# A row of 8224 bytes instead of 8192 for the weights of each step, in a gated-product kernel in float32r

## What is computed

```python
kv = np.einsum('bhsd,bhse->bhde', k, v)             # batch 4, heads 8, seq 576, head 64
out = np.einsum('bhsd,bhde->bhse', q, kv)
x = out / sqrt(mean(out * out, -1) + 1e-6) * g_norm # then as 2304 tokens x 512
h = x @ w_in;  x = (h * sigmoid(1.702 * h)) @ w_out # w_in 512 x 2048, w_out 2048 x 512
h = x @ w2_in; y = softplus(h) @ w2_out             # the same sizes
```

## Time and profile before

| what | value |
|---|---|
| median of the runs | 882.18 us (882.14 to 883.94) |
| span of the profiled execution | 881.6 us |
| outside the span, against the median | 0.6 us |
| PE (matmuls) busy | 861.9 us, 98% |
| PEld (weight loads) busy | 714.6 us, 81% |
| DVE, ACT, POOL busy | 438.1, 268.0, 205.4 us |
| matmul records | 4064 |

### The profile page before, as it was taken

How to read it: one execution, slowest core, us unless ns; L and a number is a source line. 1 busy time by engine, 2 the same in 40 slices (tenths; PEclk the granted TensorE clock), 3 DMA queues, 4 the chain that set the end, 5 groups by cost and what they waited for, 6 DMA issues and landing times.

```text
span 881.6 us, 11362 instructions
## 1 busy us (share of the span) xinstructions
PE 861.9 (98%) x4064; PEld 714.6 (81%) x4064; DVE 438.1 (50%) x769; ACT 268.0 (30%) x493; POOL 205.4 (23%) x173
## 2 busy tenths in 40 slices
PE   6999999999999999999997999999999999999997
PEld 5877888888888888888995888888888888888896
DVE  1487443433343334333587644564456445644564
ACT  3555320211021102110344433343334333433343
POOL 1459530000000000000297322132213221322132
PEclk9999999999999999999997999999999999999999
DMA  8935420000000000000052000100010001000100
GB/s 295 301 144 170 141 72 0 1 1 1 1 0 0 0 0 0 0 0 0 25 186 102 1 1 1 48 0 0 0 48 0 0 0 48 0 0 0 48 2 24
DMA packets 13868, 36.55 MB, mean 41 GB/s; under 512 B 1552, under 2 KB 3600, under 8 KB 13840
## 3 DMA queue, kind: packets, MB, share of 16 engines
q1 hardware_dynamic: 13840, 36.18, 12.0%
HBM read 31.46 MB, written 4.72 MB: 41 GB/s over the span
## 4 chain that ended last, share of the span: by engine, by line
PE 95%; DVE 2%; issue 1%; DMA 1%; ACT 1%; POOLq 0%; POOL 0%; ACTq 0%; DVEq 0%; SPq 0%
PE ps L379 44%; PE ps L407 44%; PE ps L306 3%; PE ps L317 2%; PE ps L331 1%; DMA tail_sb<-k_v 1%; DVE xs L603 1%; PE ps L343 0%; DVE gs L657 0%; DVE xy L589 0%; DVE hid L575 0%; DVE xs L605 0%; ACT sq_sb L468 0%; DVE inv_s L577 0%; DVE gs L659 0%
## 5 line engine op out<-in xcount | busy, mean ns | idle before, releaser
L657 DVE CAST gs<-hid 128x512 fp32r<-128x512 f32 (+1 forms) x160 | 76.1, 476 | 292.4 <-PE ps L407 291.0
L379 PE MATMUL ps<-xs,w_own 128*128 128x512 f32 (+1 forms) x960 | 211.2, 374 | 4.5 <-DVE xs L605 4.3
L379 PE MATMUL ps<-xs,w_shared 128*128 128x512 f32 (+1 forms) x960 | 214.7, 372 | 0.0
L379 PEld LDWEIGHTS ps<-xs,w_own 128*128 128x128 f32 x960 | 170.5, 192 | 37.8 <-DVE xs L605 6.5
L379 PEld LDWEIGHTS ps<-xs,w_shared 128*128 128x128 f32 x960 | 168.5, 188 | 35.0
L283 POOL TENSOR_TENSOR stage<-stage 128x512 f32<-128x512 f32 (+1 forms) x80 | 94.6, 1183 | 298.1 <-DVE stage L641 298.1
L513 ACT ACTIVATE hid<-ps 128x512 f32<-128x512 f32 (+1 forms) x80 | 44.5, 557 | 272.8 <-PE ps L379 250.2
L659 DVE TENSOR_TENSOR gs<-hid,gs 128x512 fp32r<-128x512 f32 (+1 forms) x160 | 115.8, 724 | 5.5
L266 POOL TENSOR_TENSOR w_own<-stage,w_own 128x512 fp32r<-128x512 f32 x32 | 42.6, 1366 | 314.8 <-ACT w_own L456 314.8
L517 ACT ACTIVATE stage<-ps 128x512 f32<-128x512 f32 (+1 forms) x80 | 44.5, 557 | 206.9 <-PE ps L379 193.0
L407 PE MATMUL ps<-gs,w_shared 128*128 128x512 f32 (+1 forms) x480 | 105.5, 373 | 0.8 <-DVE gs L657 0.6
(11 more groups left out here) (42 smaller groups left out, 443.3 us busy)
## 6 DMA issues: line engine op xcount, KB each, us to landing
stage<-moe_w SPq DMA_DIRECT2D x32, 512.0 KB, 3.3
kv_in_sb<-k_v SPq DMA_DIRECT2D x16, 512.0 KB, 5.5
q_sb<-q_t SPq DMA_DIRECT2D x16, 288.0 KB, 4.6
out<-xy SPq DMA_DIRECT2D x18, 256.0 KB, 2.2
tail_sb<-k_v SPq DMA_DIRECT2D x4, 256.0 KB, 6.0
xy<-head_bcast SPq DMA_DIRECT2D x1, 512.0 KB, 7.3
g_col<-g_norm SPq DMA_DIRECT2D x2, 0.2 KB, 6.0
```

The source lines that it names most:

```text
L379: mm = nc.tensor.matmul(bank, w[:, W_IN, wp, cols], xs[:, xp, k, 0:width], start=(k == 0 and (wp, xp) == (HI, HI)), stop=(k == KT - 1 and ...
L657: nc.vector.tensor_copy(gs[:, HI, s, :width], g).then_inc(g_hi_made, 1)
```

## The change

A step's row becomes 8224 bytes: 2056 elements, of which the last 8 are unused. `weights(f)` cuts them off and gives the same shape as before. Two unused buffers are added: one of 256 bytes behind `w_own` and one of 192 bytes ahead of the attention part's buffers and `w_shared`.

```diff
+    W_ROW = 4 * DM + 8
...
-        w_own = sb("w_own", [P, W_OWN, 2, 2, DM], F32R)
+        w_own = sb("w_own", [P, W_OWN, W_ROW], F32R)
+        sb("phase_gap", [P, 64], F32)
         xy = sb("xy", [P, KT, T], F32)
...
         eps_col = sb("eps_col", [P, 1], F32)
+        sb("phase_gap_shared", [P, 48], F32)
...
-        w_shared = sb("w_shared", [P, W_SHARED, 2, 2, DM], F32R)
+        w_shared = sb("w_shared", [P, W_SHARED, W_ROW], F32R)
...
         def weights(f):
-            return w_own[:, f] if f < W_OWN else w_shared[:, f - W_OWN]
+            row = w_own[:, f, 0:4 * DM] if f < W_OWN else w_shared[:, f - W_OWN, 0:4 * DM]
+            return row.rearrange("p (a b n) -> p a b n", a=2, b=2)
```

## The result

The changed kernel takes 887.88 us (median of five, 885.3 to 890.94) where the kernel before takes 883.0 (five runs, 882.14 to 883.94): a ratio of 1.0054, 95% interval 1.0033 to 1.0076. It is slower by 2.9 to 6.7 us. The profiled execution is the slowest of its five, 890.94 us with a span of 889.1. In all runs the time is the span and 1.8 us, so the execution profiled before, with its span of 881.6, took about 883.4, near the median of the five. What lies outside the span is 1.8 us and not the 0.6 of the prediction; by its own terms its sum should have been 884.8 + 1.8 = 886.6 us.

The account below looks back on a forecast made before the run. TensorE's rate through groups of 12 matmuls was taken as the bound. Eight chunks at +0.4 us gave +3.2, the other terms 0: 881.6 + 3.2 = 884.8, plus 0.6 outside the span 885.4, stated as 885.0 us, range 867 to 893.

Parts of the forecast that it names:

- the bounds of 88 and 89.2: Whole chunk of phase 0, forecast 88.8 us: under 88 would refute the forecast downward, over 89.2 upward.
- step (c): Whole chunks: every group meets another phase than the one before, so each takes 2.775 us; +0.4 us a chunk, +3.2 us.
- phase 0 is the exception: Rival, whole chunks: only step 0 keeps its rate, all other distances cost 2.80 us a group; 890.4 us, chance 0.17.
- (a): Steps 0 and 2: step 0 keeps phase 0, step 2 goes from 2.72 to 2.80 us a group; +0.16 us a chunk.
- (b): The other 14 steps, at unknown phases: bounds of 2.63 us (219.3 ns a matmul, from L331) and 2.80 us a group.
- (d): Chunks of 256 tokens: groups of 1.44 and 1.41 us each become 1.425; 0, with bounds of 1 us both sides.
- (e): Weight writes by ACT and POOL to new addresses: 0, range 0 to +0.7 us.
- (f): Attention buffers move together by 704 bytes; `xy`, `xs`, `stage`, `hid` and `gs` by exactly 512: 0.
- Better phases exist: Rival, whole chunks: the 14 new phases lie evenly between 2.63 and 2.80 us a group; 871.5 us, chance 0.33.
- The phase isn't the cause: Rival: the weights' memory regions set the rates, both halves keep theirs and nothing changes; 882.2 us, chance 0.10.

Follow-up runs that it names:

- `all64`: Kernel before, with unused buffers of 64 bytes ahead of `w_own` and 448 behind it, putting all 16 steps at phase 64; 887.72 us, ratio 1.0074.
- `sweep4`: Weight row of 8196 bytes and both gaps 480 bytes, so step f lies at phase 4*f; 886.03 us, one run.
- `all0`: Kernel before, with `w_shared` moved by 448 unused bytes so that all 16 steps lie at phase 0; 870.13 us, ratio to before 0.9866.
- `move64`: Weights placed modulo 512 as in `all0`, but `xs` and `gs` 64 bytes further; 889.79 us, ratio to before 1.0100.
- `all192`: Kernel before, with unused buffers around `w_own` and ahead of `w_shared` putting all 16 steps at phase 192; 889.62 us, ratio 1.0113.
- `all0_rest64`: `all0` with `xs` and `gs` used from column 48 on in the chunks of 256 tokens; 872.48 us, ratio to before 0.9879.

## Why the prediction was right or wrong

The direction, the time (885 against 887.9, in the range of 867 to 893) and the place were right: PE alone, in the matmuls' rate, with no pause and no other engine changed. The chunk of phase 0 was put at 88.8 us and takes 89.06, inside the bounds of 88 and 89.2; that of phase 1 was put at 88.5 and takes 89.13.

The mechanism was wrong in step (c). It took the groups of 2.80 and 2.75 beside each other for a cost of changing over, and so gave every group 2.775. Single phases run alone show that in phase 0 the rate is the phase's own: the kernel's chunk is their sum, 89.1 against 89.06 us, with no more than 0.1 us a chunk for the change-over. That a group of phase 0 loses something beside another phase was read rightly, but it isn't a cost that every group pays. What is true is nearly the rival *phase 0 is the exception*, which had 0.17 and 890.4 us: 12 of 16 steps run at 2.80. It was too dear by what it didn't know, the period of 256 bytes, which gives step 8 the cheap rate back, and the 2.75 of phase 192 in steps 6 and 14. Two steps at 2.72, two at 2.75 and twelve at 2.80 average 2.78, and 2.775 came near that by accident.

(a) Steps 0 and 2 came as said, 227.4 and 233.3 ns. (b) The reading of L331, that no distance among its own is free, held: at 512 columns none of the distances tried is under 226.7, so its low end of 219.3 ns was never met, and the top of 2.80 us was passed a little, by 234.6 ns in the changed kernel. At 256 columns the low end does occur: 113.3 ns in `all64` is 6.6 above the 106.7 of the columns, near the 6 of L331's shortest. (d) The chunk of 256 in phase 0 stayed, 48.49 to 48.42 us. (e) POOL's writes are at 1368 and 1415 ns instead of 1366 and 1412, ACT's with them: 0. (f) `xs`, `gs` and the rest: 0; the way to the first `up` took 0.7 us more, 65.3 us, less than what the other kernels differ by (62.5 to 64.7 us), but above the highest of them.

*Better phases exist* (0.33) is out at 512 columns: over the 16 phases of the change and the 16 of `sweep4`, none beats 0. At 256 columns it holds, 46.93 us for the chunk in `all64` against 48.49, too little to pay for the whole chunks. *The phase isn't the cause* (0.10) is out by `all0`, `all64` and `move64`, and with it, for these matmuls, the rule of the Trainium skill that TensorE's reads take nothing from each other ("TensorE: Matmul & The Clock Gate", Part 2): by that rule `all0` would be at 883 us and not at 870. Phase 1 was worse than forecast, +1.0 us a chunk, because `down` there had rates of 228.9 to 230.3 in most of steps 8 to 15, at distance +64, and in the changed kernel only steps 2 and 10 have that distance and 229.9.

## What to carry to other kernels

Where TensorE is the bound and loads weights beside each matmul, compare the time from group to group for tiles of different buffers; if they differ with the same shapes, look at where the operands lie modulo 256 bytes. For matmuls of 512 columns, lay the weights and the moving operand so that all their tiles start at the same place modulo 256 (a pad of 448 bytes gave 1.3% here), and don't let row pads or small constants between buffers shift one against the other. At 256 columns the same place was among the dearest, 120.0 ns against 113.3 to 117.8 at distance 64, so there measure before you pad. Read the rate in the steady middle of each stretch and not from the total, which also holds how the handovers fell.

## What the runs showed of the hardware

- In phase 0, matmuls in float32r of 512 columns with a weight load each take 226.7 ns at distance 0 and 256 bytes, 227.3 at 16, 228.9 at 192, and 231.3 to 234.6 at 32, 64, 96, 128 and 224. At 2.4 GHz the columns are 213.3 ns.
- The sign counts: with the stationary operand 64 bytes further than the moving one, modulo 256, 233.3 ns in `all64`; with the moving one 64 bytes further, 228.9 in phase 0 of `all192`, though up to 233.3 in `up` of its phase 1.
- The rates are exact and repeat to a tenth of a ns or two, and more than one can belong to a distance: 113.3 and 117.8 ns at 256 columns and distance 64, 228.9, 230.3 and 233.3 in `up` of `all192`'s phase 1, 226.7 and 231.2 at distance 0 beside groups of 512 and of 256 columns.
- One DVE cast of 64x288 took 0.5 to 1.4 us in eleven kernels and 6.3 and 6.7 in two, each time until 0.16 to 0.17 us behind the end of a POOL subtraction, and 0.43 us on ACT.
- After the handover to phase 1, in which TensorE waits, the granted clock fell to 1.2 GHz for about 3.6 us in `all0` and 10 us before and in `all0_rest64`; the start of the phase was 2 us shorter in `all0`.
